# The matrix engine's waits thinned out and spread over products, in an attention and two-layer MLP kernel

## The chip, the cores and the metric

One core of one Trainium2 chip. The time is that of the device for one execution of the program, in microseconds (us); the median of three runs is compared. TensorE is the matrix engine, with a sequencer that reads its instructions; VectorE, ScalarE (ACT in the profile) and GpSimd (POOL) are the others, and SyncE (SP) issues most transfers.

## The reference

```python
# attention, per batch and head; q, k, v: (2, 8, 768, 64), block 32, window 16
k_sum = k.reshape(B, H, nb, 32, D).max(axis=3)
v_sum = v.reshape(B, H, nb, 32, D).mean(axis=3)
scores = concat([where(|i - j| < 16, scale * q @ k.T, -1e9), scale * q @ k_sum.T + log(32)])
attn = softmax(scores) @ concat([v, v_sum])
# first layer: x is attn as 1536 tokens x 512
x = relu(x @ w_in) ** 2 @ w_out                 # 512 -> 2048 -> 512
# second layer
h = x @ w2_in                                   # 512 -> 1024
solu = h * softmax(h)
out = ((solu - mean) / sqrt(var + 1e-6) * g_ln) @ w2_out    # 1024 -> 512
```

## The kernel before

**Precision.** The MLP products are made in three passes (`PASSES`): every operand is split into a high and a low part of a fast 32-bit format, and high x high, high x low and low x high are added up. So each 128 x 128 tile of weights takes three products on TensorE.

**Attention** is cut into 32 units `u`. A unit is a pair of heads (`p = u % 4`) and 192 query rows (three tiles of 64, `TPU`). Three steps of TensorE belong to it. `scores(u)` multiplies queries with the 24 block maxima and the window of 96 keys (12 small products in the profile, L805); VectorE masks them into `probs` (`masked_ok`), ScalarE takes exponentials, VectorE normalises (`norm_ok`). `turned(u)` transposes the three tiles (L818), and ScalarE copies them to `probsT` (`probsT_ok`). `values(u)` multiplies with the block means and the value window (12 products, L852); ScalarE and VectorE split the result into `x_hi` and `x_lo` (`xlo_ok`). GpSimd cuts the windows of keys for `scores` (`kwin_ok`) and copies the block maxima beside them (`kbc_ok`).

**The first layer** runs over 64 steps `n`, 16 per chunk of 384 tokens. `up(n)` makes one 128-wide slice of the hidden layer in four parts `k` of three products (L863); ScalarE and VectorE make relu, square and the split. `down(n)` adds it to the four output slices `d`, three products each (L892). Each takes about 2.08 us of TensorE.

**The order is written out by hand.** Units 0 to 8 are the head: a list of calls in `tensor` up to `scores(9)`. Behind it, the loop over `n` has two halves `j` per step, `up(n + 2)` at an even and `down(n)` at an odd half. `SLOTS` names the 24 halves ahead of which the three steps of attention stand: `values(a)`, `turned(a + 1)`, `scores(a + 2)`. Each such place is called a slot below.

**The second layer** runs over 12 tiles of 128 tokens, in a loop `s` of 14 rounds. A round has `h2(s)` (24 products of 512 columns, L988, two halves of four parts `k`), the transposes of tile s - 1 (8, L1003), and the output products of tile s - 2 (24, L1015). Between them VectorE and ScalarE make, for tile s: maximum (L754), exponential, `solu` (L762, `solu_ok`), `cen` (L769, `cen_ok(s + 1)`: the wait for tile s - 1 is `cen_ok >= s`), and, for tile s - 1 and behind `cen` in VectorE's order, the low part `lnT_lo` (L775, `lnlo_ok >= s`). In round 0 the last two down-projections stand behind `h2(0)`.

**Waits.** `pe.wait_ge(sem, value)` holds the next instruction of TensorE until a semaphore has a value. One wait rides on the product itself. Further ones become instructions of their own in front of it (EVENT_SEMAPHORE, on the sequencer, "PEldq" in the profile), which hold up all that follows. A wait stands at each of the groups named: all of a group's waits are written ahead of its first product, as in

```python
                    pe.wait_ge(cen_ok, s)
                    if s == 1:
                        pe.wait_ge(yclo_ok, KD * (NCHUNK - 1) + 2)
                    else:
                        pe.wait_ge(lnlo_ok, s - 1)
                    for f in range(F2):
```

Of the kernel before, what the change touches and what calls it, by code (L numbers as in the profile page):

```python
# [23 lines left out]
PPB = H // 2  # L24
# [5 lines left out]
KD = DM // P  # L30
F1 = FF1 // P
F2 = FF2 // P
FH = FF2 // 512
CH = 384
NCHUNK = TOK // CH
XC = KD * CH
TT = TOK // P
TPC = CH // P
# [6 lines left out]
HPC = CH // UQ  # L45
UNITS = B * RB * PPB
UPB = RB * PPB
UPC = HPC * PPB
# [28 lines left out]
def build(nc, qT, q_head, kT, vrows, vblk, vwin, vwin_head, w_in_t, w_out_t, w2_t, g_cols, mask_c, ident_c, y_dram, out):  # L77
    ctx = ExitStack()
    with ctx:
# [705 lines left out]
        def _(pe):  # L785
# [2 lines left out]

            def scores(u):
                row, p = u // PPB, u % PPB  # L790
                if u < UPC:
                    pe.wait_ge(qf_in[row], 16)
                else:
                    pe.wait_ge(q_in[p], 16 * (row - HPC + 1))
                pe.wait_ge(kwin_ok, u + 1)
                pe.wait_ge(kbc_ok, (u // UPB) * PPB + p + 1)
                if u >= UPC:
                    pe.wait_ge(masked_ok, u)
                elif u >= 2:
                    pe.wait_ge(masked_ok, u - 1)  # L800
                out_ = scores_bank(u)
                for t in range(TPU):
                    for e in range(2):
                        rows = slice(e * D, (e + 1) * D)
                        last = nc.tensor.matmul(out_[e * QT:(e + 1) * QT, t * KX:(t + 1) * KX],  # L805
                                                q_tile(u, rows, t),
                                                k_ext[rows, p, t * KX:(t + 1) * KX],
                                                start=True, stop=True, skip_group_check=True)
                last.then_inc(scores_ok, 1)

            def turned(u):
                pe.wait_ge(norm_ok, u + 1)
                if u >= UPC:
                    pe.wait_ge(probsT_ok, u)
                elif u >= 2:
                    pe.wait_ge(probsT_ok, u - 1)
                for t in range(TPU):
                    last = nc.tensor.transpose(turned_bank(u, t), probs[:, u % 2, t * KX:(t + 1) * KX], ident[:, 0:P])  # L818
                last.then_inc(probsT_ps, 1)

# [12 lines left out]
            def values(u):  # L833
                row, p = u // PPB, u % PPB
                if u < UPC:
                    pe.wait_ge(vwf_in[row], 16)
                    pe.wait_ge(vmean_ok, p + 1)
                elif u < UPB:
                    pe.wait_ge(vw_in[p], 16 * (row - HPC + 1))
                    pe.wait_ge(vkept_ok, 1)  # L840
                else:
                    pe.wait_ge(vw_in[p], 16 * (row - HPC + 1))
                    pe.wait_ge(vs_in[p], 16)
                pe.wait_ge(probsT_ok, u + 1)
                if u >= UPC:
                    pe.wait_ge(xlo_ok, u)
                elif u >= 2:
                    pe.wait_ge(xlo_ok, u - 1)
                out_ = xT_bank(u)
                for t in range(TPU):  # L850
                    for e in range(2):
                        last = nc.tensor.matmul(out_[e * D:(e + 1) * D, t * QT:(t + 1) * QT],  # L852
                                                v_tile(u, t, e),
                                                probsT[0:KX, u % 2, t * P + e * QT:t * P + (e + 1) * QT],
                                                start=True, stop=True, skip_group_check=True)
                last.then_inc(attn_ps, 1)

            def up_part(n, k):
                c, f = n // F1, n % F1
                if f == 0:  # L860
                    pe.wait_ge(xlo_ok, c * UPC + (HPC - 1) * PPB + k + 1)
                for a, b in PASSES:
                    last = nc.tensor.matmul(up_bank(n), win[a][:, f * WC + k * P:f * WC + (k + 1) * P],  # L863
                                            x[b][:, c % 2, k * CH:(k + 1) * CH],
                                            start=(k == 0 and a == 0 and b == 0), stop=(k == KD - 1 and a == 1),
                                            skip_group_check=True)
                if k == KD - 1:
                    last.then_inc(up_ok, 1)
# [14 lines left out]
            def down(n):  # L883
                c, f = n // F1, n % F1
                if c == 0:
                    pe.wait_ge(wout_lo_ok, f + 1)
                pe.wait_ge(hlo_ok, n + 1)
                for d in range(KD):
                    if f == 0 and c:
                        pe.wait_ge(yclo_ok, KD * (c - 1) + d + 1)  # L890
                    for a, b in PASSES:
                        last = nc.tensor.matmul(down_bank(d), wout[a][:, f * WC + d * P:f * WC + (d + 1) * P],  # L892
                                                h[b][:, n % 3, :],
                                                start=(f == 0 and a == 0 and b == 0),
                                                stop=(f == F1 - 1 and a == 1), skip_group_check=True)
                last.then_inc(down_ok, 1)
# [66 lines left out]
            def y_tile(i, a, k):  # L963
# [2 lines left out]
                at = k * CH + (i % TPC) * P  # L966
                return x[a][:, (i // TPC) % 2, at:at + P]

            for s in range(TT + 2):
                p = s % 2  # L970
                if s < TT:
                    if s == 0:
                        pe.wait_ge(w2_lo_ok, KD * FH)
                        pe.wait_ge(masked_ok, UNITS)
                        pe.wait_ge(probsT_ok, UNITS)
                        pe.wait_ge(xlo_ok, UNITS)
                    if s == 1:
                        pe.wait_ge(relu_ok, STEPS)
                    if s >= 2:
                        pe.wait_ge(solu_ok, s - 1)  # L980
                    if s < (NCHUNK - 2) * TPC:
                        pe.wait_ge(y_in[p], 32 * (s // 2 + 1))
                    else:
                        pe.wait_ge(yclo_ok, KD * (s // TPC + 1))
                    for half in range(FH):
                        for k in range(KD):
                            for a, b in PASSES:
                                last = nc.tensor.matmul(bank[:, (0, 6)[p] + half, :], y_tile(s, a, k),  # L988
                                                        w2[b][:, (k * FH + half) * WC:(k * FH + half + 1) * WC],
                                                        start=(k == 0 and a == 0 and b == 0),  # L990
                                                        stop=(k == KD - 1 and a == 1))
                    last.then_inc(h2_ok, 1)
                if s == 0:
                    down(STEPS - 2)
                    down(STEPS - 1)
                if 1 <= s <= TT:
                    pe.wait_ge(cen_ok, s)
                    if s == 1:
                        pe.wait_ge(yclo_ok, KD * (NCHUNK - 1) + 2)
                    else:  # L1000
                        pe.wait_ge(lnlo_ok, s - 1)
                    for f in range(F2):
                        last = nc.tensor.transpose(bank[:, 2 + f // 4, (f % 4) * P:(f % 4 + 1) * P],  # L1003
                                                   cen[:, 1 - p, f * P:(f + 1) * P], ident[:, 0:P])
                    last.then_inc(lnT_ps, 1)
                if s >= 2:
                    if s == 2:
                        pe.wait_ge(w2_lo_ok, F1)
                        pe.wait_ge(yclo_ok, KD * NCHUNK)
                    if s >= 4:  # L1010
                        pe.wait_ge(o_ok, s - 3)
                    pe.wait_ge(lnlo_ok, s - 1)
                    for f in range(F2):
                        for a, b in PASSES:
                            last = nc.tensor.matmul(bank[:, 4 + p, :], ln[a][:, p, f * P:(f + 1) * P],  # L1015
                                                    w2[b][:, (F2 + f) * WC:(F2 + f + 1) * WC],
                                                    start=(f == 0 and a == 0 and b == 0),
                                                    stop=(f == F2 - 1 and a == 1))
                    last.then_inc(o_ps, 1)
# [66 lines left out]
```

## Time and profile before

| | |
|---|---|
| median of 3 runs | 493.81 us (493.63 to 494.09) |
| the profiled execution | 493.39 us |
| its span | 491.6 us |
| TensorE products busy | 482.8 us, 98% of the span, 3144 products |
| TensorE weight loads busy | 436.3 us (89%), beside the products |
| VectorE, ScalarE, GpSimd busy | 253.3, 210.1, 29.4 us |
| TensorE's granted clock | full over the whole span |

The span is the time from the first to the last instruction; the rest of the execution's 493.39 us lies around it. Times in the views count from the start of the span. A product is pipelined: its recorded length is longer than the distance from one to the next, so the distance of starts is what it costs. Weight loads (PEld) run ahead beside the products before them where they can.

### The profile page before, as it was taken

Reading aid. Unit: us, or ns where it says so; the run is one execution under the profiler, and the core shown is the slowest. Engines: PE = TensorE matmul, PEld = TensorE weight load, DVE = VectorE, ACT = ScalarE, POOL = GpSimd, SP = SyncE. Lnnn points to the kernel's source line nnn. Section 1 sums busy time; section 2 is a strip of 40 time slices with the busy share of each in tenths; the row PEclk is TensorE's granted clock in tenths of the full one; section 3 lists DMA queues with packets and bytes.
Section 4 is the critical chain, followed back from the end, with each engine's and each line's share of the span. In section 5 each row is a group of like instructions: output and inputs, shape, how many; then the busy total and the mean of one; then the engine's idle time right before and its main releaser. Section 6 shows DMA issues by size and latency. Waiting matters only on the chain.

```text
span 491.6 us, 8265 instructions
## 1 busy us (share of the span) xinstructions
PE 482.8 (98%) x3144; PEld 436.3 (89%) x3144; DVE 253.3 (52%) x511; ACT 210.1 (43%) x549; POOL 29.4 (6%) x61
## 2 busy tenths in 40 slices
PE   8979999999999999999999999999999999999997
PEld 6869898999999999999999999999888888888885
DVE  4878767885544444544443244446674444444440
ACT  2877666554443433544334233334443333333341
POOL 2230000211000000000000000000000000000000
PEclk9999999999999999999999999999999999999999
DMA  8998132120400001320000321212132000000001
GB/s 301 331 363 277 58 106 87 53 73 16 167 21 22 21 21 41 108 63 20 21 2 1 87 86 43 87 43 87 43 87 64 23 21 23 21 24 38 27 22 43
DMA packets 26679, 37.39 MB, mean 76 GB/s; under 512 B 2480, under 2 KB 16592, under 8 KB 26640
## 3 DMA queue, kind: packets, MB, share of 16 engines
q1 hardware_dynamic: 25808, 34.60, 21.7%
q10 hardware_dynamic: 832, 2.27, 1.3%
q8 instruction: 25, 0.41, 0.4%
q14 instruction: 14, 0.11, 0.1%
HBM read 30.41 MB, written 6.29 MB: 75 GB/s over the span
## 4 chain that ended last, share of the span: by engine, by line
PE 94%; DVE 3%; DMA 1%; ACT 1%; issue 1%; POOL 0%; DVEq 0%; ACTq 0%; POOLq 0%
PE bank L863 28%; PE bank L892 27%; PE bank L1015 12%; PE bank L988 12%; PE bank L805 5%; PE bank L818 3%; PE bank L852 3%; PE bank L1003 2%; PE bank L829 1%; DMA k_raw<-kT 1%; DVE solu L762 1%; DVE stat L754 1%; DVE lnT_lo L775 0%; DVE k_sum L591 0%; DVE cen L769 0%
## 5 line engine op out<-in xcount | busy, mean ns | idle before, releaser
L863 PE MATMUL bank<-x_hi,win_hi 128*128 128x384 f32 x256 | 88.2, 345 | 0.0
L892 PE MATMUL bank<-h_hi,wout_hi 128*128 128x384 f32 x256 | 86.0, 336 | 0.0
L863 PE MATMUL bank<-x_hi,win_lo 128*128 128x384 f32 x256 | 85.7, 335 | 0.0
L892 PE MATMUL bank<-h_hi,wout_lo 128*128 128x384 f32 x256 | 85.7, 335 | 0.0
L863 PE MATMUL bank<-x_lo,win_hi 128*128 128x384 f32 x256 | 85.7, 335 | 0.0
L892 PE MATMUL bank<-h_lo,wout_hi 128*128 128x384 f32 x256 | 85.6, 334 | 0.0
L643 DVE TENSOR_TENSOR sqr<-relu 128x384 f32<-128x384 f32 x64 | 35.9, 561 | 89.0 <-ACT relu L477 88.6
L477 ACT ACTIVATE relu<-bank 128x384 f32<-128x384 f32 x64 | 31.5, 492 | 109.0 <-PE bank L863 109.0
L863 PEld LDWEIGHTS bank<-x_hi,win_hi 128*128 128x128 f32 x256 | 48.0, 188 | 3.2 <-issue 3.0
L892 PEld LDWEIGHTS bank<-h_hi,wout_hi 128*128 128x128 f32 x256 | 48.1, 188 | 0.7 <-issue 0.5
L892 PEld LDWEIGHTS bank<-h_lo,wout_hi 128*128 128x128 f32 x256 | 48.1, 188 | 0.0
L863 PEld LDWEIGHTS bank<-x_lo,win_hi 128*128 128x128 f32 x256 | 48.1, 188 | 0.0
L863 PEld LDWEIGHTS bank<-x_hi,win_lo 128*128 128x128 f32 x256 | 48.1, 188 | 0.0
L892 PEld LDWEIGHTS bank<-h_hi,wout_lo 128*128 128x128 f32 x256 | 48.0, 188 | 0.0
L754 DVE TENSOR_REDUCE stat<-bank 128x1 f32<-128x1024 f32 x12 | 14.7, 1224 | 49.1 <-PE bank L988 49.1
L564 ACT ACTIVATE e_sb<-bank,stat 128x1024 f32<-128x1024 f32 x12 | 13.4, 1117 | 61.3 <-DVE stat L754 61.3
L423 ACT ACTIVATE probs<-probs,neg_max 128x120 f32<-128x120 f32 x96 | 36.5, 383 | 6.6 <-DVE neg_max L619 6.6
L1015 PE MATMUL bank<-win_hi,lnT_hi 128*128 128x512 f32 x96 | 38.4, 400 | 0.0
L647 DVE TENSOR_TENSOR h_lo<-sqr,h_hi 128x384 fp32r<-128x384 f32 x64 | 35.8, 560 | 4.6 <-DVE sqr L643 0.4
L1015 PE MATMUL bank<-win_hi,lnT_lo 128*128 128x512 f32 x96 | 37.5, 390 | 0.0
L1015 PE MATMUL bank<-win_lo,lnT_hi 128*128 128x512 f32 x96 | 37.4, 389 | 0.0
L481 ACT ACTIVATE h_hi<-relu 128x384 fp32r<-128x384 f32 x64 | 33.7, 527 | 2.0
(80 smaller groups left out, 705.8 us busy)
## 6 DMA issues: line engine op xcount, KB each, us to landing
win_raw<-w_in_t SPq DMA_DIRECT2D x8, 512.0 KB, 12.5
wout_raw<-w_out_t SPq DMA_DIRECT2D x8, 512.0 KB, 13.4
win_raw<-w_t SPq DMA_DIRECT2D x8, 512.0 KB, 3.3
v_ext<-vwin SPq DMA_DIRECT2D x24, 144.0 KB, 3.3
out<-o_sb SPq DMA_DIRECT2D x12, 256.0 KB, 2.0
k_raw<-kT SPq DMA_DIRECT2D x7, 400.0 KB, 4.3
q_sb<-qT SPq DMA_DIRECT2D x24, 96.0 KB, 3.1
v_next<-vblk SPq DMA_DIRECT2D x4, 384.0 KB, 3.4
```

The source lines that it names most:

```text
L423: last = nc.scalar.activation(probs[:, s, c], probs[:, s, c], ACT.Exp, bias=neg_max[:, s, t:t + 1], accum_out=row_sum[:, s, t:t + 1])
L477: nc.scalar.activation(relu[:, n % 2, :], up_bank(n), ACT.Relu).then_inc(relu_ok, 1)
L481: nc.scalar.activation(h_hi[:, n % 3, :], relu[:, n % 2, :], ACT.Square).then_inc(hhi_ok, 1)
L643: nc.vector.tensor_tensor(sqr[:, n % 3, :], relu[:, n % 2, :], relu[:, n % 2, :], ALU.mult)\
L647: nc.vector.tensor_tensor(h_lo[:, n % 3, :], sqr[:, n % 3, :], h_hi[:, n % 3, :].bitcast(F32), ALU.subtract).then_inc(hlo_ok, 1)
L754: nc.vector.tensor_reduce(stat[:, p, 0:1], h2_bank(s), AX.X, ALU.max, negate=True).then_inc(m2_ok, 1)
L805: last = nc.tensor.matmul(out_[e * QT:(e + 1) * QT, t * KX:(t + 1) * KX], q_tile(u, rows, t), k_ext[rows, p, t * KX:(t + 1) * KX], start=T ...
L818: last = nc.tensor.transpose(turned_bank(u, t), probs[:, u % 2, t * KX:(t + 1) * KX], ident[:, 0:P])
L863: last = nc.tensor.matmul(up_bank(n), win[a][:, f * WC + k * P:f * WC + (k + 1) * P], x[b][:, c % 2, k * CH:(k + 1) * CH], start=(k == 0 a ...
L892: last = nc.tensor.matmul(down_bank(d), wout[a][:, f * WC + d * P:f * WC + (d + 1) * P], h[b][:, n % 3, :], start=(f == 0 and a == 0 and b ...
L988: last = nc.tensor.matmul(bank[:, (0, 6)[p] + half, :], y_tile(s, a, k), w2[b][:, (k * FH + half) * WC:(k * FH + half + 1) * WC], start=(k ...
L1015: last = nc.tensor.matmul(bank[:, 4 + p, :], ln[a][:, p, f * P:(f + 1) * P], w2[b][:, (F2 + f) * WC:(F2 + f + 1) * WC], start=(f == 0 and ...
```

## The change

Three things. Waits that another one implies are dropped (for instance the `masked_ok` wait of `scores` from unit 9 on, the window wait of all but the first unit of a row in the head). Of those that stay, some are moved to a product in front of the group, so that each product carries one: the value window and `xlo_ok` of a slot onto parts 2 and 3 of the half before it (`slot_ahead`), the query load onto the second transpose of `turned` (`queries`), and in the second layer `cen_ok`, `lnlo_ok` and `o_ok` onto parts 1, 2 and 3 of the second half of `h2(s)`, `solu_ok` and the `y` wait onto the last two parts of the output products of the round before. And where several stay at one place, their order is another: in the head `turned` now names `probsT_ok` before `norm_ok`, and `scores` names `kwin_ok` last.

```diff
--- before.py
+++ after.py
@@ -788,16 +788,16 @@
 
             def scores(u):
                 row, p = u // PPB, u % PPB
-                if u < UPC:
+                if u < UPC and p == 0:
                     pe.wait_ge(qf_in[row], 16)
-                else:
-                    pe.wait_ge(q_in[p], 16 * (row - HPC + 1))
+                if u % UPB < PPB:
+                    pe.wait_ge(kbc_ok, (u // UPB) * PPB + p + 1)
+                if u == UPC:
+                    queries(u)
+                if 2 <= u <= UPC:
+                    pe.wait_ge(masked_ok, u - 1)
+
                 pe.wait_ge(kwin_ok, u + 1)
-                pe.wait_ge(kbc_ok, (u // UPB) * PPB + p + 1)
-                if u >= UPC:
-                    pe.wait_ge(masked_ok, u)
-                elif u >= 2:
-                    pe.wait_ge(masked_ok, u - 1)
                 out_ = scores_bank(u)
                 for t in range(TPU):
                     for e in range(2):
@@ -808,13 +808,19 @@
                                                 start=True, stop=True, skip_group_check=True)
                 last.then_inc(scores_ok, 1)
 
+            def queries(u):
+                pe.wait_ge(q_in[u % PPB], 16 * (u // PPB - HPC + 1))
+
             def turned(u):
+                if 2 <= u < UPC:
+                    pe.wait_ge(probsT_ok, u - 1)
+
+                if u == UPC:
+                    pe.wait_ge(probsT_ok, u)
                 pe.wait_ge(norm_ok, u + 1)
-                if u >= UPC:
-                    pe.wait_ge(probsT_ok, u)
-                elif u >= 2:
-                    pe.wait_ge(probsT_ok, u - 1)
                 for t in range(TPU):
+                    if t == 1 and UPC < u + 1 < UNITS:
+                        queries(u + 1)
                     last = nc.tensor.transpose(turned_bank(u, t), probs[:, u % 2, t * KX:(t + 1) * KX], ident[:, 0:P])
                 last.then_inc(probsT_ps, 1)
 
@@ -833,19 +839,16 @@
             def values(u):
                 row, p = u // PPB, u % PPB
                 if u < UPC:
-                    pe.wait_ge(vwf_in[row], 16)
+                    if p == 0:
+                        pe.wait_ge(vwf_in[row], 16)
                     pe.wait_ge(vmean_ok, p + 1)
-                elif u < UPB:
-                    pe.wait_ge(vw_in[p], 16 * (row - HPC + 1))
+                    if u >= 2:
+                        pe.wait_ge(xlo_ok, u - 1)
+                elif u == UPC:
                     pe.wait_ge(vkept_ok, 1)
-                else:
-                    pe.wait_ge(vw_in[p], 16 * (row - HPC + 1))
+                elif UPB <= u < UPB + PPB:
                     pe.wait_ge(vs_in[p], 16)
                 pe.wait_ge(probsT_ok, u + 1)
-                if u >= UPC:
-                    pe.wait_ge(xlo_ok, u)
-                elif u >= 2:
-                    pe.wait_ge(xlo_ok, u - 1)
                 out_ = xT_bank(u)
                 for t in range(TPU):
                     for e in range(2):
@@ -855,8 +858,18 @@
                                                 start=True, stop=True, skip_group_check=True)
                 last.then_inc(attn_ps, 1)
 
+            def slot_ahead(h, k):
+
+                if h + 1 in SLOTS:
+                    u = SLOTS[h + 1][0]
+                    if k == 2:
+                        pe.wait_ge(vw_in[u % PPB], 16 * (u // PPB - HPC + 1))
+                    if k == 3:
+                        pe.wait_ge(xlo_ok, u)
+
             def up_part(n, k):
                 c, f = n // F1, n % F1
+                slot_ahead(2 * n - 4, k)
                 if f == 0:
                     pe.wait_ge(xlo_ok, c * UPC + (HPC - 1) * PPB + k + 1)
                 for a, b in PASSES:
@@ -888,6 +901,7 @@
                 for d in range(KD):
                     if f == 0 and c:
                         pe.wait_ge(yclo_ok, KD * (c - 1) + d + 1)
+                    slot_ahead(2 * n + 1, d)
                     for a, b in PASSES:
                         last = nc.tensor.matmul(down_bank(d), wout[a][:, f * WC + d * P:f * WC + (d + 1) * P],
                                                 h[b][:, n % 3, :],
@@ -966,6 +980,17 @@
                 at = k * CH + (i % TPC) * P
                 return x[a][:, (i // TPC) % 2, at:at + P]
 
+            def h2_ahead(s):
+
+                if s >= 2:
+                    pe.wait_ge(solu_ok, s - 1)
+
+            def y_ahead(s):
+                if s < (NCHUNK - 2) * TPC:
+                    pe.wait_ge(y_in[s % 2], 32 * (s // 2 + 1))
+                else:
+                    pe.wait_ge(yclo_ok, KD * (s // TPC + 1))
+
             for s in range(TT + 2):
                 p = s % 2
                 if s < TT:
@@ -976,14 +1001,18 @@
                         pe.wait_ge(xlo_ok, UNITS)
                     if s == 1:
                         pe.wait_ge(relu_ok, STEPS)
-                    if s >= 2:
-                        pe.wait_ge(solu_ok, s - 1)
-                    if s < (NCHUNK - 2) * TPC:
-                        pe.wait_ge(y_in[p], 32 * (s // 2 + 1))
-                    else:
-                        pe.wait_ge(yclo_ok, KD * (s // TPC + 1))
+                    if s < 3:
+                        h2_ahead(s)
+                        y_ahead(s)
                     for half in range(FH):
                         for k in range(KD):
+
+                            if half == 1 and k == 1 and s >= 2:
+                                pe.wait_ge(cen_ok, s)
+                            if half == 1 and k == 2 and s >= 2:
+                                pe.wait_ge(lnlo_ok, s - 1)
+                            if half == 1 and k == 3 and s >= 4:
+                                pe.wait_ge(o_ok, s - 3)
                             for a, b in PASSES:
                                 last = nc.tensor.matmul(bank[:, (0, 6)[p] + half, :], y_tile(s, a, k),
                                                         w2[b][:, (k * FH + half) * WC:(k * FH + half + 1) * WC],
@@ -994,10 +1023,11 @@
                     down(STEPS - 2)
                     down(STEPS - 1)
                 if 1 <= s <= TT:
-                    pe.wait_ge(cen_ok, s)
                     if s == 1:
+                        pe.wait_ge(cen_ok, s)
                         pe.wait_ge(yclo_ok, KD * (NCHUNK - 1) + 2)
-                    else:
+                    elif s == TT:
+                        pe.wait_ge(cen_ok, s)
                         pe.wait_ge(lnlo_ok, s - 1)
                     for f in range(F2):
                         last = nc.tensor.transpose(bank[:, 2 + f // 4, (f % 4) * P:(f % 4 + 1) * P],
@@ -1007,10 +1037,16 @@
                     if s == 2:
                         pe.wait_ge(w2_lo_ok, F1)
                         pe.wait_ge(yclo_ok, KD * NCHUNK)
-                    if s >= 4:
+                    if s >= TT:
                         pe.wait_ge(o_ok, s - 3)
-                    pe.wait_ge(lnlo_ok, s - 1)
+                    if s == TT + 1:
+                        pe.wait_ge(lnlo_ok, s - 1)
                     for f in range(F2):
+
+                        if f == F2 - 2 and s + 1 < TT:
+                            h2_ahead(s + 1)
+                        if f == F2 - 1 and s + 1 < TT:
+                            y_ahead(s + 1)
                         for a, b in PASSES:
                             last = nc.tensor.matmul(bank[:, 4 + p, :], ln[a][:, p, f * P:(f + 1) * P],
                                                     w2[b][:, (F2 + f) * WC:(F2 + f + 1) * WC],
```

## Rows read from the trace of the kernel before

**Rows 1.** The page: TensorE's busy time and the chain by engine.

```profile
PE 482.8 (98%) x3144; PEld 436.3 (89%) x3144; DVE 253.3 (52%) x511; ACT 210.1 (43%) x549; POOL 29.4 (6%) x61
...
PE 94%; DVE 3%; DMA 1%; ACT 1%; issue 1%; POOL 0%; DVEq 0%; ACTq 0%; POOLq 0%
```

**Rows 2.** Busy time by stage; columns: stage, its length, each engine.

```profile
0.00:44.00 44.00, 38.90 (x377) 31.33 (x378) 29.34 (x70) 27.83 (x96) 11.20 (x27) 1.00 1.00 327
44.00:364.00 320.00, 319.86 (x2182) 302.01 (x2181) 172.96 (x352) 140.53 (x391) 12.56 (x24) 1.00 0.18 58
364.00:470.00 106.00, 106.00 (x505) 88.43 (x504) 44.93 (x82) 35.43 (x54) 5.12 (x10) 1.00 0.10 33
470.00:491.60 21.60, 18.08 (x86) 14.55 (x84) 6.05 (x10) 6.31 (x9) 0.55 (x1) 1.00 0.10 37
```

**Rows 3.** Order of time, TensorE, the slot at 142 us; columns: start, length.

```profile
141.60 0.34 PE L892 MATMUL bank<-h_hi,wout_lo 128*128 128x384 f32 x1
141.87 0.57 PE L852 MATMUL bank<-probsT,v_ext 120*64 120x64 f32 x12
...
142.84 0.83 PE L805 MATMUL bank<-k_ext,q_sb 64*64 64x120 f32 x12
143.60 0.44 PE L863 MATMUL bank<-x_hi,win_hi 128*128 128x384 f32 x1
```

**Rows 4.** A sequencer wait of that slot: ns min/median/max, first and last start.

```profile
L798 PEldq EVENT_SEMAPHORE  x1: 51/51/51, 142.0 to 142.0; - x1
```

**Rows 5.** Order of time on TensorE, the slot at 52 us.

```profile
52.45 0.83 PE L805 MATMUL bank<-k_ext,q_sb 64*64 64x120 f32 x12
53.21 0.45 PE L892 MATMUL bank<-h_hi,wout_hi 128*128 128x384 f32 x1
```

**Rows 6.** Order of time, TensorE, a down-projection that carries four waits.

```profile
207.46 0.33 PE L892 MATMUL bank<-h_hi,wout_hi 128*128 128x384 f32 x1
...
209.37 0.33 PE L892 MATMUL bank<-h_hi,wout_lo 128*128 128x384 f32 x1
```

**Rows 7.** Order of time: the latest `x_lo` ahead of a slot, that slot.

```profile
210.74 0.35 DVE L636 TENSOR_TENSOR x_lo<-bank,x_hi 128x192 fp32r<-128x192 f32 x1
...
213.79 0.57 PE L852 MATMUL bank<-probsT,v_ext 120*64 120x64 f32 x12
```

**Rows 8.** The chain in the head, then two rows of the timeline.

```profile
9.69 0.14 issue
...
30.81 0.04 issue
...
31.43 0.48 ACT L432 COPY probsT<-bank 120x384 f32<-120x384 f32 x1 [0.42 <-PE bank L818]
...
32.17 0.57 PE L852 MATMUL bank<-probsT,v_ext_first 120*64 120x64 f32 x12 [0.20 <-ACT probsT L432]
```

**Rows 9.** Order of time, second layer, round s = 5.

```profile
392.39 1.22 DVE L775 TENSOR_TENSOR lnT_lo<-bank,lnT_hi 128x1024 fp32r<-128x1024 f32 x1
...
397.49 0.39 PE L988 MATMUL bank<-win_hi,y_hi 128*128 128x512 f32 x1
```

**Rows 10.** Order of time, second layer, round s = 2.

```profile
361.11 0.39 PE L988 MATMUL bank<-win_hi,y_hi 128*128 128x512 f32 x1
...
361.42 0.76 DVE L769 TENSOR_SCALAR cen<-solu,stat 128x1024 f32<-128x1024 f32 x1
...
362.09 1.22 DVE L775 TENSOR_TENSOR lnT_lo<-bank,lnT_hi 128x1024 fp32r<-128x1024 f32 x1
...
362.92 0.39 PE L988 MATMUL bank<-win_hi,y_lo 128*128 128x512 f32 x1
...
363.45 1.07 PE L1003 MATMUL bank<-ident,cen 128*128 128x128 f32 x8
...
364.27 0.48 PE L1015 MATMUL bank<-win_hi,lnT_hi 128*128 128x512 f32 x1
...
364.59 0.39 PE L1015 MATMUL bank<-win_lo,lnT_hi 128*128 128x512 f32 x1
```

## The prediction, made before the changed kernel was run

> **What bounds the kernel now.** I read the page first. TensorE is busy for 98% of the span at a full clock, and the chain that ended last lies on it for 94% [rows 1]. So time can be won or lost only where TensorE waits. The view by stages says where that is: 5.1 us in the attention head (0 to 44 us), 0.14 us from 44 to 364, and 3.5 us behind 470, beside the last tile and the final stores; in between there is none [rows 2].
>
> Then I looked up the waits that stand as instructions of their own on TensorE's sequencer. One lasts 51 ns [rows 4], and over all of TensorE's lines I count 231. Their lines are never that of a group's first wait: a product carries the one written first, and each one or two of the others make such an instruction. By that rule I count 148 that go: 48 of `values`, 23 of `turned`, 49 of `scores`, 28 of the second layer. The question is whether the sequencer ever holds up the products.
>
> **The slots (24 of them, 44 to 339 us): nothing.** A slot is values, turned, scores. Around 142 us the last separate wait of `scores` ran at 142.0, 0.8 us ahead of its products at 142.84, and those of `values` ran further ahead still [rows 3, 4]. Still each change of shape costs something: 0.27 us from the last wide product to `values` instead of 0.17. Is that the waits' doing? From `scores` to the next wide product it is the same 0.76 us where that wide product has a separate wait (52.45 to 53.21, the down-projection's weights still being split) and where it has only a carried one (142.84 to 143.60) [rows 3, 5]. So the gap comes with the change of shape, and the removed instructions are worth nothing where the sequencer is ahead.
>
> What the slots gain instead are carried waits in the stream in front: the v window on the third quarter and `x_lo` on the fourth, three products apart. Down-projections at a chunk's start carry four waits three products apart already, and their step is 0.173 us throughout (207.46 to 209.37 is eleven steps) [rows 6]. Are the signals there by then? The latest is `x_lo` after a chunk's first unit: done at 211.09, wanted three products ahead of 213.79, that is at 213.2 [rows 7]. The v windows go out three or four slots ahead. So they cost nothing. One wait sits closer: the q load is waited for on the second of the three transposes of `turned`, one product behind the carried wait of the first, 23 times. No row shows two carried waits that close. Nearest below is the 3-product distance, at 0 [rows 6]; nearest above a separate wait at the front, 0.10 us (next part), so 0 to 2.3 us in all. I take 0, since the load is long there and three products hold no trace of a loss.
>
> **The head (0 to 44 us): about nothing.** Here the sequencer is at the front, and the chain gives the price. A signal that ends a carried wait is followed by the product in 0.04 us (30.81). One that ends a separate wait takes 0.14 us (9.69), and one with two separate ones 0.26 us (ACT's copy ends at 31.91, the product starts at 32.17) [rows 8]. So each separate wait at the front is 0.10 us, each second one 0.11. The change moves four of these:
> - `scores(1)`: `kbc_ok`, the late one, is now written first and carried: 0.14 becomes 0.04, a gain of 0.10.
> - `turned(6)` and `turned(8)`: for u = 2 to 8 the `probsT_ok` wait is now written ahead of `norm_ok`, so the late `norm_ok` becomes the separate one: 0.04 becomes 0.14, a loss of 0.10 each. Both lie on the chain.
> - `values(6)`: two separate waits become one, a gain of 0.11.
>
> The sum is -0.10 + 0.20 - 0.11 = -0.01 us. `scores(8)` waits for POOL's window copy with the same separate wait before and after. `scores(4)` to `scores(7)` and `values(5)` lose a separate wait each, and nothing waits for them: what they gain ends in ScalarE's busy queue or that POOL copy. I keep -0.2 to +0.2 for this part.
>
> **The second layer, tile loop s = 2: +1.33 us.** This is where the change costs. Before, `cen_ok` and `lnlo_ok` stood behind all 24 products of `h2(s)`, ahead of the transposes. For every s from 2 to 11 they now stand inside `h2(s)`: `cen_ok(s)` on product 16 of 24, `lnlo_ok(s-1)` on product 19. From s = 3 on that is free. In the round at 393 us `lnT_lo`, the later of the two, ended at 393.61, and product 19 would want it only at 397.49: 3.9 us of room [rows 9]. At s = 2 the pipeline is still filling: tile 1's `cen` ends at 362.18, and tile 0's `lnT_lo`, behind it in VectorE's order, ends at 363.31. In the trace product 16 starts at 361.11 (so product 19 at 361.79), the last at 362.92, and TensorE then idles till the transposes at 363.45 [rows 10]. That small idle was all the late signals cost, since the products stood ahead of the wait.
>
> With the waits inside: product 16 waits from 361.11 to 362.22. Three products follow (0.32 with its weights exposed, as at 364.27 to 364.59, then 0.227 each, an eighth of the way from 361.11 to 362.92), up to 362.99. Product 19 waits for `lnlo_ok`, so it starts at 363.31 + 0.04 = 363.35. Six products follow: 0.32 + 5 x 0.227 = 1.46, so the transposes start at 364.81 against 363.45, 1.36 us later. They get about 0.03 back, their first weights now being loaded ahead: 1.33. What was work beside a wait is now work behind it.
>
> Does anything later swallow this? VectorE's work on tile 2 starts when the last product of `h2(2)` is done, and that moves by 1.66 us (362.92 to 364.58), 0.3 more than the rest. So at s = 3 the room of 3.9 us shrinks by 0.3, and no more; from 364 to 470 us TensorE has no gap that could take up the rest [rows 2]. The tail (the last tile's vector chain, transposes, 24 products, store) hangs on the end of `h2(11)`, so it only shifts. The other 28 removed waits of this layer ran ahead; the waits for `solu_ok` and `y_in` now ride on the last quarter of the products in front, their signals many products old. These are worth 0.
>
> **Sum.** 0 - 0.01 + 1.33 = +1.32 us. The profiled execution took 493.39 us (span 491.6), which makes 494.7; the median of the runs, 493.81, stands 0.42 above it, so I forecast **495.1 us** for the median. A measurement of this kernel can tell about 0.2%, 1.0 us, from no change, so the forecast lies just outside it.
>
> **Rivals.**
> - *The separate waits do cost in the slots, so faster.* Each slot has three places where one goes. At 0.05 us each, half the head's price, 24 x 3 x 0.05 = 3.6 us less, 493.81 - 3.6 + 1.32 = 491.5 us. For it: 0.27 instead of 0.17 us at every entry of a slot, and idle put down to no releaser. Against it: equal gaps with and without. It decides from 0.03 us a place on (2.3 us). Chance 0.12. A weaker form, 0.01 us a place (0.7 us), ends at 494.4, no change: 0.08. The Trainium skill (Advanced Engine Details and Errata, Network/Comms) puts the reading of a semaphore by a sequencer at 50 to 100 ns; 148 such reads, all on the path, would be an estimated 7 to 15 us less. By it the time would be 480 to 488 us. The 51 ns of a separate wait agree with the size, not with its lying on the path.
> - *Slower still.* The q wait on the second transpose cannot enter until the first has begun, so its weights are loaded late: up to 0.10 us x 23 = 2.3 us, at 0.05 us 1.2 us, which makes 496.3, at most 497.4 us. For it: only one product lies between the two. Against it: carried waits three apart are free. Chance 0.13.
> - *The move does not bite at s = 2.* A carried wait might hold up less than I think, or VectorE might be earlier: 493.8 us. Against it: the signals' times come from VectorE's own order, which the change does not touch. Chance 0.05.
>
> **Numbers.** The forecast has 0.62, and its own range is 494.6 to 495.6: 0.54 of it over 0.2%, 0.08 below. Slower is 0.54 + 0.13 = 0.67, no change 0.08 + 0.08 + 0.05 = 0.21, faster 0.12. The range reaches down to take in the two cases of no change and up to most of the slower one: 493.7 to 496.8; the faster case stays out.
>
> **What would show it.** Right: in `h2(2)` a hole of about 1.1 us ahead of product 16 and one of 0.4 ahead of product 19, transposes at 364.8, everything behind shifted alike; slots with the same 0.27, 0.97 and 0.76 us into `values`, from there to `scores`, and on to the wide product; 83 separate waits where there were 231; `turned(6)` 0.14 us behind its signal. Wrong: a slot that is shorter from `values` to the wide product than 1.73 us, a way from `values` to `scores` longer than 0.97 us, or h2(2) without a hole.

## The result, and the profile after

The changed kernel takes 494.91 us (median of 17 runs, 494.55 to 496.66), the kernel before, run beside it, 493.68 us (17 runs, 493.44 to 494.42). The ratio is 1.0024, with a 95% interval of 1.0018 to 1.0030: +1.2 us, just over the 0.2% that counts as a difference here. The forecast was 495.1 us.

The page of the changed kernel, its head, TensorE's busy time and the chain by engine:

```profile
span 493.8 us, 8117 instructions
...
PE 483.9 (98%) x3144; PEld 437.0 (89%) x3144; DVE 253.1 (51%) x511; ACT 210.1 (43%) x549; POOL 29.4 (6%) x61
...
PE 94%; DVE 3%; DMA 1%; ACT 1%; issue 1%; POOL 0%; DVEq 0%; ACTq 0%; POOLq 0%
```

There are 148 instructions fewer (8265 before, 8117 now), and the kernel is slower all the same. TensorE is as busy as before, and the chain is on it for the same 94% [rows 1]. The profiled execution took 495.57 us with a span of 493.8, more than most of this kernel's runs (spans of 492.7 to 493.4 in 14 of the 17), because TensorE's granted clock fell for some microseconds in the head; the last section shows the row. A second profile of the same kernel (`after_again`, below) has a full clock and a span of 492.9 us, and is used where positions are compared.

Busy time by stage of the first profile (columns: stage, its length, each engine's busy time, TensorE's granted clock, DMA):

```profile
0.00:44.00 44.00, 38.71 (x363) 31.45 (x363) 28.18 (x68) 27.05 (x94) 11.19 (x27) 0.96 1.00 318
44.00:364.00 320.00, 319.04 (x2185) 300.85 (x2183) 173.04 (x352) 141.14 (x392) 12.18 (x23) 1.00 0.19 60
364.00:470.00 106.00, 105.83 (x504) 88.29 (x503) 45.58 (x83) 35.63 (x56) 5.50 (x10) 1.00 0.10 33
470.00:493.80 23.80, 20.28 (x97) 16.41 (x95) 6.25 (x10) 6.31 (x9) 0.55 (x1) 1.00 0.09 34
```

Against [rows 2]: the middle stretch, 44 to 364 us, now holds 1.0 us without a product (320.0 less 319.04) where there was 0.14, and the next one 0.17 where there was none. Round s = 2 of the second layer lies at its end. In order of time there, in the second profile (columns: start, length, engine, line, operation, idle time before it and what ended it):

```profile
361.43 0.75 DVE L769 TENSOR_SCALAR cen<-solu,stat 128x1024 f32<-128x1024 f32 x1
362.09 1.22 DVE L775 TENSOR_TENSOR lnT_lo<-bank,lnT_hi 128x1024 fp32r<-128x1024 f32 x1
...
362.24 0.50 PE L1017 MATMUL bank<-win_hi,y_hi 128*128 128x512 f32 x1 [0.96 <-DVE cen L769]
...
363.37 0.50 PE L1017 MATMUL bank<-win_hi,y_hi 128*128 128x512 f32 x1 [0.17 <-DVE lnT_lo L775]
...
364.86 1.03 PE L1033 MATMUL bank<-ident,cen 128*128 128x128 f32 x8
```

This answers to [rows 10]. Product 16 of `h2(2)` stands at 362.24 where it stood at 361.11, right behind `cen`; product 19 at 363.37, right behind `lnT_lo`; the transposes at 364.86 instead of 363.45. VectorE's two operations are where they were, to 0.01 us. The last product of the program then begins at 489.27 us:

```profile
489.27 0.39 PE L1051 MATMUL bank<-win_hi,lnT_lo 128*128 128x512 f32 x1
```

It began at 487.91 before: 1.36 us, all of it there since round s = 2. (That the positions ahead of round 2 agree to 0.01 us is partly chance. The first load of keys took 4.45 us in this execution and 4.30 before, so that `scores(0)`, which itself gained 0.05, began 0.10 us later, at 6.57 instead of 6.47, and the rest of the head won that much back. Counted from `scores(0)`, the last product comes 1.26 us later.) The slot at 142 us, in the same profile, is that of [rows 3] to 0.01 us:

```profile
141.88 0.57 PE L855 MATMUL bank<-probsT,v_ext 120*64 120x64 f32 x12
142.38 0.54 PE L824 MATMUL bank<-ident,probs 128*120 128x128 f32 x3
142.85 0.83 PE L805 MATMUL bank<-k_ext,q_sb 64*64 64x120 f32 x12
143.61 0.44 PE L876 MATMUL bank<-x_hi,win_hi 128*128 128x384 f32 x1
```

And the chain in the head (first profile) shows the waits that were moved there (columns: start, length, what; "issue" lies between a signal and the product that waited for it):

```profile
9.93 0.04 issue
...
27.63 0.14 issue
...
31.65 0.14 issue
...
32.83 0.13 issue
...
36.86 0.14 issue
```

These are `scores(1)`, `scores(8)`, `turned(6)`, `values(6)` and `turned(8)`. In [rows 8] the first has 0.14, `turned(6)` 0.04, and `values(6)` begins 0.26 us behind ScalarE's copy.

### The profile page after: what moved, and what is told of

Read it like the earlier page. It is cut to its first block, busy times and chain, and to the rows that moved or that the text cites. A ratio compares the mean times of both kernels' runs of the same rounds, so it can differ in the third digit from the quotient of the medians.

```text
span 493.8 us, 8117 instructions
## 1 busy us (share of the span) xinstructions
PE 483.9 (98%) x3144; PEld 437.0 (89%) x3144; DVE 253.1 (51%) x511; ACT 210.1 (43%) x549; POOL 29.4 (6%) x61
## 4 chain that ended last, share of the span: by engine, by line
PE 94%; DVE 3%; DMA 1%; ACT 1%; issue 1%; POOL 0%; DVEq 0%; ACTq 0%; POOLq 0%
PE bank L876 27%; PE bank L906 27%; PE bank L1017 12%; PE bank L1051 12%; PE bank L805 5%; PE bank L824 3%; PE bank L855 3%; PE bank L1033 2%; PE bank L835 1%; DMA k_raw<-kT 1%; DVE solu L762 1%; DVE stat L754 1%; DVE lnT_lo L775 0%; DVE k_sum L591 0%; DVE cen L769 0%
```

## The experiments

Eight kernels ran, in two groups of four, each group beside its own runs of the kernel before (medians 493.77 and 493.86 us). The theory was: the removed waits are worth nothing, the head evens out, and the whole difference is two waits inside `h2(2)`. The rivals were that separate waits cost something in the slots, and that the loss lies elsewhere and only shows from s = 2 on.

**One part undone: round 2 back as it was.** The changed kernel, but with both waits of s = 2 behind the 24 products again:

```diff
-                            if half == 1 and k == 1 and s >= 2:
+                            if half == 1 and k == 1 and s >= 3:
                                 pe.wait_ge(cen_ok, s)
-                            if half == 1 and k == 2 and s >= 2:
+                            if half == 1 and k == 2 and s >= 3:
                                 pe.wait_ge(lnlo_ok, s - 1)
...
-                    elif s == TT:
+                    elif s in (2, TT):
                         pe.wait_ge(cen_ok, s)
                         pe.wait_ge(lnlo_ok, s - 1)
```

> The changed kernel, with the two waits of round s = 2 (cen_ok, lnlo_ok) put back behind h2(2), ahead of the transposes; all else as changed. Theory (the whole loss is round 2): 1.35 us less than the changed kernel, so 493.6 us, the same as before within 0.2; h2(2) without a hole, transposes 0.53 us behind its last product. Rival (the loss is spread: the q wait on the second transpose, waits in the stream): 494.5 us or more, and h2(2) mended all the same.

Measured: 493.74 us (12 runs), ratio 1.0000 [0.9991, 1.0009]. In order of time:

```profile
361.20 0.39 PE L1017 MATMUL bank<-win_hi,y_hi 128*128 128x512 f32 x1
...
362.18 1.22 DVE L775 TENSOR_TENSOR lnT_lo<-bank,lnT_hi 128x1024 fp32r<-128x1024 f32 x1
...
363.01 0.39 PE L1017 MATMUL bank<-win_hi,y_lo 128*128 128x512 f32 x1
...
363.55 1.06 PE L1033 MATMUL bank<-ident,cen 128*128 128x128 f32 x8
```

No hole; TensorE idles only behind the last product (363.01), until 0.15 us after `lnT_lo` (362.18 + 1.22). The loss is gone with one edit in one round, while 147 of the 148 separate waits stay away. (The two waits together at the transposes make one of them separate again.) So the other parts of the change add up to nothing that the medians can tell. In the traces they are worth about 0.1 us, all of it in the head: from `scores(0)` to the last product it is 481.44 us before and 481.36 here.

**One part alone: only round 2, on the kernel before.** The reverse: all 231 separate waits kept, and only these four lines added to `h2`:

```diff
                         for k in range(KD):
+                            if half == 1 and k == 1 and s == 2:
+                                pe.wait_ge(cen_ok, s)
+                            if half == 1 and k == 2 and s == 2:
+                                pe.wait_ge(lnlo_ok, s - 1)
```

> The kernel before, with one thing of the change: in round s = 2 cen_ok also on product 16 and lnlo_ok on product 19 of h2(2). The 148 separate waits stay. Theory: the whole loss, 1.35 us: 495.0 us. Rival (the 148 removed waits give something back that the changed kernel's total hides): the loss here is larger than the changed kernel's 1.23 by what they give, 0.3 us or more: 495.3 or above against the changed kernel's 494.9 beside it.

Measured: 495.05 us (11 runs), ratio 1.0018 [1.0007, 1.0028]. On TensorE, in order of time, with the last product of the program at the end:

```profile
362.27 0.50 PE L992 MATMUL bank<-win_hi,y_hi 128*128 128x512 f32 x1 [0.96 <-DVE cen L769]
...
363.40 0.50 PE L992 MATMUL bank<-win_hi,y_hi 128*128 128x512 f32 x1 [0.17 <-DVE lnT_lo L775]
...
364.90 1.03 PE L1007 MATMUL bank<-ident,cen 128*128 128x128 f32 x8
...
489.31 0.39 PE L1019 MATMUL bank<-win_hi,lnT_lo 128*128 128x512 f32 x1
```

Within 0.04 us these are the changed kernel's positions. Two waits in one round are enough for the whole loss: from the start of `cen` in that round to the last product it is 126.49 us before and in `e1_s2_back`, 127.84 in `after_again` and 127.85 here. Counted from `scores(0)` it is 482.78 us here and 482.70 in `after_again`; the difference is the head's gain.

**Which of the two waits costs it?** First only `cen_ok` inside `h2(2)`, with `lnlo_ok` behind it:

```diff
-                            if half == 1 and k == 2 and s >= 2:
+                            if half == 1 and k == 2 and s >= 3:
                                 pe.wait_ge(lnlo_ok, s - 1)
...
+                    elif s == 2:
+                        pe.wait_ge(lnlo_ok, s - 1)
```

> The changed kernel, with only cen_ok left on product 16 of h2(2), and lnlo_ok behind h2(2). Theory: products 16 to 24 start at cen's end: 0.34 + 8 x 0.227 = 2.16 us later the transposes may start, which is later than lnlo_ok by 1.0 us, so the loss is 0.9 to 1.0 us: 494.5 us. Rival (each hole adds its own share, the 1.12 of the cen hole and 0.34 + 0.1 of the other): 1.1 to 1.2 us, 494.75.

Measured: 494.77 us (8 runs), ratio 1.0027 [1.0017, 1.0037].

```profile
361.83 0.75 DVE L769 TENSOR_SCALAR cen<-solu,stat 128x1024 f32<-128x1024 f32 x1
362.50 1.22 DVE L775 TENSOR_TENSOR lnT_lo<-bank,lnT_hi 128x1024 fp32r<-128x1024 f32 x1
...
362.64 0.50 PE L1017 MATMUL bank<-win_hi,y_hi 128*128 128x512 f32 x1 [0.96 <-DVE cen L769]
...
363.45 0.40 PE L1017 MATMUL bank<-win_hi,y_hi 128*128 128x512 f32 x1
...
364.84 1.04 PE L1035 MATMUL bank<-ident,cen 128*128 128x128 f32 x8
```

The hole ahead of product 16 is there, the one ahead of product 19 is not (363.45 follows in step). This execution's round lies late: `cen` starts at 361.83 where it was 361.43, since the first load of keys took 4.84 us instead of 4.45. Counted from `cen`'s start, the transposes come 3.01 us later; in the kernel without a hole (`e1_s2_back`, `cen` at 361.51) it was 2.04, in the kernel with both (`after_again`) 3.43. So one wait costs 0.97 us and both cost 1.39. `cen_ok` at product 16 leaves nine products behind it, 2.2 us of work (362.64 to 364.84); `lnT_lo` ends beside them and no longer matters.

Then only `lnlo_ok`, on product 19, with `cen_ok` behind `h2(2)` (the mirror image of the edit above):

```diff
-                            if half == 1 and k == 1 and s >= 2:
+                            if half == 1 and k == 1 and s >= 3:
                                 pe.wait_ge(cen_ok, s)
...
+                    elif s == 2:
+                        pe.wait_ge(cen_ok, s)
```

> The changed kernel, with only lnlo_ok left on product 19 of h2(2), and cen_ok behind h2(2). Theory: only the later signal counts with the products behind it, so the loss is the same 1.35 us as with both: 494.9 us, with one hole of 1.5 us ahead of product 19. Rival (the cen hole is the main part, 1.12 of 1.35): about 0.3 us, 494.0.

Measured: 494.92 us (11 runs), ratio 1.0020 [1.0012, 1.0029].

```profile
361.56 0.39 PE L1017 MATMUL bank<-win_hi,y_lo 128*128 128x512 f32 x1
362.08 1.22 DVE L775 TENSOR_TENSOR lnT_lo<-bank,lnT_hi 128x1024 fp32r<-128x1024 f32 x1
...
363.36 0.50 PE L1017 MATMUL bank<-win_hi,y_hi 128*128 128x512 f32 x1 [1.41 <-DVE lnT_lo L775]
...
364.85 1.03 PE L1035 MATMUL bank<-ident,cen 128*128 128x128 f32 x8
```

One gap of 1.8 us from start to start (361.56 to 363.36) in place of the two, and the transposes at 364.85, as with both waits. So the losses don't add: what counts is the later signal plus the products that stand behind its wait. With `lnlo_ok` inside, `cen_ok` costs nothing more. The whole-run medians (+1.0 and +1.15 us) are too near each other to tell the two kernels apart; the traces do it.

**What is a separate wait worth in a slot?** Removing them brought nothing; how many could be added? On the kernel before, more waits on signals given long ago are written ahead of `scores(u)` for u over 8. Two signals make one more separate wait, so eight make four more ahead of each of 23 groups, the 22 slots that hold a `scores` and `scores(9)` at the end of the head:

```diff
+            LONG_DONE = [(ident_in, 16), (mask_in, 16), (edge_in, 16), (qf_in[0], 16), ...
...
+                if u > UPC:
+                    for done, value in LONG_DONE[:8]:
+                        pe.wait_ge(done, value)
                 out_ = scores_bank(u)
```

> The kernel before, with four more separate waits (two long-given signals each) ahead of scores(u) from u = 9 on: 92 more waits in 23 slots. Theory (the sequencer is 0.8 us ahead there and one wait takes it 0.11 us): 0.44 us of its lead used, no time lost: 493.7 us. Rival (a separate wait costs time in a slot, 0.05 us each): 92 x 0.05 = 4.6 us more, 498.3.

Measured: 493.92 us (12 runs), ratio 1.0003 [0.9991, 1.0015]. A slot of it:

```profile
143.09 0.57 PE L860 MATMUL bank<-probsT,v_ext 120*64 120x64 f32 x12
143.59 0.54 PE L826 MATMUL bank<-ident,probs 128*120 128x128 f32 x3
144.06 0.83 PE L813 MATMUL bank<-k_ext,q_sb 64*64 64x120 f32 x12
144.83 0.44 PE L871 MATMUL bank<-x_hi,win_hi 128*128 128x384 f32 x1
```

0.50, 0.47 and 0.77 us from one to the next, the kernel before's numbers, with six separate waits ahead of `scores` instead of two. With 24 signals, twelve more waits each (276 in all), it was expected to show:

> The same with twelve more ahead of each scores(u): 276 more waits. Theory (lead of 0.73 us, 0.108 us a wait): 1.30 us are needed, 0.57 us are missing in each of 23 slots, 13 us more: 507 us. Rival (0.05 us each from the first on): 276 x 0.05 = 13.8 us as well, so this one tells them apart only beside the run with four; if it costs under 3 us, a wait takes the sequencer less than 0.07 us.

Measured: 507.06 us (4 runs), ratio 1.0254 [1.0235, 1.0272]. A slot, and then the separate waits ahead of its `scores` (count, ns, first and last start):

```profile
148.85 0.57 PE L860 MATMUL bank<-probsT,v_ext 120*64 120x64 f32 x12
149.35 0.54 PE L826 MATMUL bank<-ident,probs 128*120 128x128 f32 x3
150.38 0.83 PE L813 MATMUL bank<-k_ext,q_sb 64*64 64x120 f32 x12 [0.49 <-issue]
```

```profile
L808 PEldq EVENT_SEMAPHORE  x14: 51/51/51, 148.9 to 150.3; - x14
```

Only the way from `turned` to `scores` has grown: 1.03 us instead of 0.47 here, 1.04 in the median of the 22 slots. Added up over these slots it is 12.8 us more, and `scores(9)` starts 1.02 us behind the last wide product instead of 0.28. Together that is 13.5 us, where the medians differ by 13.2. The fourteen waits begin with the first product of `values` (148.9 and 148.85) and come every 0.108 us (thirteen steps in 1.4 us). They take 1.51 us, where `scores` stands 0.97 us behind `values` in a slot without delay: 0.54 too much. Two waits take 0.22 of the 0.97 and six 0.65, so neither shows. (That these waits begin with `values` is read from the traces, and holds for `scores` alone; see the last section.) Separate waits in a slot do have a price, but it is paid only once that lead is used up, and the change went from two to none.

**The late signal written first.** The changed kernel with round 2 put back (as in the first experiment), and the late signal of each group in the head named first, so that the product carries it:

```diff
             def turned(u):
+                pe.wait_ge(norm_ok, u + 1)
                 if 2 <= u < UPC:
                     pe.wait_ge(probsT_ok, u - 1)
...
-                pe.wait_ge(norm_ok, u + 1)
```

and likewise `probsT_ok` at the front of `values`, `kwin_ok` at that of `scores(8)`.

> The kernel of e1, and in the head the signal that comes last is written first, so that it is the carried one: norm_ok in turned, probsT_ok in values, kwin_ok in scores(8). Theory (a separate wait at the front costs 0.10 us, a carried one nothing): turned(6) and turned(8) 0.10 less each, values(6) 0.10, scores(8) 0.10: 0.4 us less than e1, 493.2 us, and the chain's issue pieces there 0.04 where they were 0.14. Rival (the head's end is set by transfers or by ScalarE's queue, not by the waits): the same as e1.

Measured: 493.52 us (11 runs), ratio 0.9997 [0.9989, 1.0006]: not to be told from the kernel before. The chain, however, shows each term:

```profile
27.91 0.04 issue
...
30.36 0.82 DVE probs L630
31.18 0.04 issue
...
36.25 0.04 issue
```

`scores(8)`, `turned(6)` and `turned(8)` now follow their signals by 0.04 us, where the changed kernel had 0.14. From `scores(0)` to `turned(8)` the head takes 29.36 us, against 29.62 in the first experiment: 0.26 us less, not the 0.4 expected. Four places were to gain 0.10 each. Counted from `scores(0)`, `scores(8)` begins 0.07 us earlier, and the steps from there to `turned(6)`, on to `values(6)` and on to `turned(8)` are shorter by 0.03, 0.07 and 0.09. At `scores(8)` the copy itself ends 0.03 later. At `turned(6)` two operations of VectorE, the small one at L625 and the multiply at L630 that gives `norm_ok(7)`, took 0.16 and 0.81 us here and 0.39 and 0.53 in `e1_s2_back`, 0.05 us more together. Four copies on GpSimd ran beside them, from 29.25 to 30.78 here:

```profile
29.25 1.53 POOL L368 COPY k_ext<-k_raw 128x288 f32<-128x288 f32 x4
```

The same copies ran from 28.93 to 30.46 in `e1_s2_back`. So in each kernel the operation that was long lay beside the copies, but the short one of 0.16 us did too, and whether the copies stretch them was not tried by itself.

**The changed kernel once more**, for a profile with a full clock and a second median.

> The changed kernel again, beside the others of this call. 494.9 us. It tells whether the dip of TensorE's clock in the head, seen in the profiled execution, comes back.

Measured: 495.11 us (12 runs), ratio 1.0018 [1.0006, 1.0029]. Its rows are those of the first section. The two measurements of the changed kernel, 1.0024 and 1.0018, agree; both lie about the 0.2% bound, and a single one would not place it above.

## Why the prediction was right

- **The separate waits in the slots: nothing.** Right. Over the 22 slots that have all three steps (the last two of the 24 have no `scores`), the medians of the ways into `values`, on to `turned`, to `scores` and to the wide product are 0.27, 0.50, 0.47 and 0.76 us in the kernel before, in the changed one, and in `e1_s2_back`, `e4_late_first` and `e5_four_more`. The rival "faster" (491.5 us) falls, its weak form too: with all waits kept (`e7_only_s2`) the loss is that of the changed kernel, and with 92 more nothing happens. The runs with added waits show the reason behind the argument from equal gaps: the sequencer has some 0.75 us in hand (0.97 less the 0.22 of two waits). The Trainium skill (Advanced Engine Details and Errata, Network/Comms) puts a semaphore read at 50 to 100 ns; 51 ns recorded and 0.108 us from one to the next are near that size, but the estimate made with it, 480 to 488 us, missed by about 7 us or more. Such a price shows in the time only where the sequencer is at the front.
- **The carried waits put in front of the slots, and the q wait on the second transpose: nothing.** Right. This was the part with the widest bounds (0 to 2.3 us), and no row showed two carried waits one product apart. The way from `turned` to `scores`, which holds the second and third transpose, is 0.47 us as before. The "slower still" rival (496.3 to 497.4) falls with it.
- **The head: -0.01 us.** Right within the margin of 0.2 us that it was given, and nearly right in each term that was counted. `scores(1)` won 0.10, `turned(6)` and `turned(8)` lost 0.10 each, `values(6)` won 0.12 instead of 0.11. Three terms were missed. `scores(8)`, said to keep its wait, follows POOL's copy by 0.14 us instead of 0.09; `scores(0)` follows its signal by 0.09 instead of 0.14; and `turned(5)` begins 0.09 later, which is hidden, since `scores(8)` then waits for that copy anyway. From `scores(0)` to `turned(8)` it is 29.60 us in `after_again` and 29.64 before. To the first slot, at 43.30 in both traces, it is 36.73 and 36.83. So the head gains 0.10 us there.
- **Round s = 2: +1.33 us.** Right: predicted 362.22, 363.35 and 364.81 for product 16, product 19 and the transposes, measured 362.24, 363.37 and 364.86. At the end of the program it is +1.36. Of the 0.05 us at the transposes, 0.02 come from the step behind the signal (0.06 us, where 0.04 was taken from the head) and 0.03 from the six products behind it (1.49 instead of 1.46). The transposes then give 0.03 back, as predicted (0.82 us to the next product before, 0.79 now). Counted from `cen` to the last product, the loss is 1.35 us, so nothing later swallowed or added to it.
- **The sum.** +1.32 predicted; +1.23 and +1.25 as differences of medians, +1.36 between traces at a full clock, of which 0.10 is the later `scores(0)`: counted from there it is +1.26, the 1.35 of round 2 less the head's 0.1. What separates that from the +1.32 is the head's gain, which was not foreseen, less the 0.02 us by which round 2 came out larger. The "does not bite" rival (493.8) falls.
- What the prediction didn't see is which of the two waits carries the loss. It walked through both and left the impression that two holes (1.1 and 0.4 us) make it up. `e3_lnlo_in` shows that `lnlo_ok` alone gives all of it.

## What to carry to other kernels

A wait moved ahead in the stream, so that each product carries one, turns every product behind it into work that can no longer be done beside the wait. It is free only if the signal is older than that distance in every round, the ones in which the pipeline fills among them: here rounds 3 to 11 cost nothing (round 5 had 3.9 us of room), and round 2 alone cost 1.3 us. What it saves must be read first: separate waits cost only where the sequencer has no lead on the products, and there it is as good to write the latest signal first, so that the product itself carries it.

## What the runs showed of the hardware

**How far ahead the sequencer is.** The separate waits ahead of `scores` start with the first product of `values`, in the kernel before too: at 141.9 and 142.0, with `values` at 141.87 [rows 3, 4]. So a slot's lead is the 0.97 us from `values` to `scores`, less what the waits there take. Each takes 0.108 us, although the trace records 51 ns of it. It could look as if the carried wait of `values` held the sequencer until that group begins, but the same slot speaks against it. These are a separate wait of `values`, the one of `turned` and one of `scores`:

```profile
L844 PEldq EVENT_SEMAPHORE  x1: 51/51/51, 138.7 to 138.7; - x1
...
L814 PEldq EVENT_SEMAPHORE  x1: 51/51/51, 140.8 to 140.8; - x1
...
L796 PEldq EVENT_SEMAPHORE  x1: 51/51/51, 141.9 to 141.9; - x1
```

The wait of `turned` is written behind all twelve products of `values`, and it ran 1.07 us before the first of them began. So the sequencer had gone past the carried wait of `values`. At the waits of `values` and at that of `turned` 17 or 18 products written ahead of them had not begun, at that of `scores` only 13 to 15. What sets these distances no run here shows.

**The clock fell in the head, in some executions.** Granted clock in the first profile of the changed kernel (columns as above, the clock ahead of the last two):

```profile
26.00:28.00 2.00, 0.56 (x12) 0.36 (x8) 1.70 (x5) 1.43 (x7) 2.00 (x3) 0.96 1.07 296
28.00:32.00 4.00, 3.60 (x50) 3.02 (x48) 1.41 (x5) 1.93 (x9) 2.51 (x5) 0.59 1.06 373
```

TensorE had stood idle from 26.4 to 27.8 us, waiting for GpSimd's key window. Then the clock was 0.59 of full speed over four microseconds, a mean of the two levels, 1.2 and 2.4 GHz, near the lower one. The twelve products of `scores(8)` took 1.42 us instead of 0.83. The last product comes 0.84 us later than in `after_again`. Of that, 0.13 was there at `scores(0)` already, and 0.71 is what the clock cost. In `after_again` TensorE stands idle as long at that place (1.44 us by its recorded rows in both), and its clock stays at 1.00 over 28 to 32 us. A kernel built from the code before, `e5_four_more`, shows the same as the changed one, for longer:

```profile
28.00:32.00 4.00, 3.24 (x52) 2.82 (x52) 2.10 (x9) 2.05 (x9) 2.86 (x5) 0.79 1.06 378
32.00:36.00 4.00, 4.00 (x39) 3.18 (x37) 2.17 (x5) 2.23 (x9) 0.00 (x0) 0.78 1.05 387
```

The runs of the kernel before beside it bear this out: 20 of 29 have a mean clock of 0.999 or more and took 493.56 to 493.99 us, and nine have 0.993 or 0.997 and took 494.58 to 495.99. So it does not belong to the change, and positions are best compared between traces that both have a full clock there. Runs with a mean clock of 0.999 or more alone give the same reading: medians of 493.79 us for the kernel before, 495.11 for the changed one and 495.05 for `e7_only_s2`, all three of one group.
